# The four-token sums of the first half batch, computed by GpSimd between its weight pieces in place of VectorE

## What is computed

```python
B, H, S, D = 4, 8, 576, 64
q_d = q.reshape(B, H, S // 4, 4, D).mean(axis=3)      # likewise k_d, v_d
out_up = np.repeat(softmax_attention(q_d, k_d, v_d), 4, axis=2)
scores = where(abs(i - j) < 4, (q @ k.T) / 8, -1e9)
out_local = softmax(scores) @ v
x = (out_up + out_local)  # as 2304 tokens x 512
h = x @ w_in              # 512 -> 2048
x = where(h > 0, h, exp(min(h, 0)) - 1) @ w_out       # 2048 -> 512
g = x @ w_gate            # 512 -> 1536
out = (g * sigmoid(g) * (x @ w_val)) @ w_out2
```

## Time and profile before

| | us |
|---|---|
| three runs | 1067.14, 1067.51, 1065.35 |
| median | 1067.14 |
| span of the profiled execution | 1064.6 |
| TensorE busy in it | 1020.6 (96%) |
| VectorE, ScalarE, GpSimd busy in it | 492.5, 383.6, 179.7 |

### The profile page before, as it was taken

The page is one execution under the profiler, slowest core; times in us unless marked ns, Lnnn a source line. Parts: engine busy times, 40 slices in busy tenths (PEclk is TensorE's granted clock), DMA queues, the critical chain, the costliest instruction groups (busy, mean ns, idle before and its releaser), DMA issues.

```text
span 1064.6 us, 20019 instructions
## 1 busy us (share of the span) xinstructions
PE 1020.6 (96%) x7136; PEld 990.1 (93%) x7136; DVE 492.5 (46%) x1459; ACT 383.6 (36%) x1204; POOL 179.7 (17%) x207
## 2 busy tenths in 40 slices
PE   5499999899999999999999999999999999999998
PEld 4389999799998899999999999999999999999998
DVE  7856576365674555755644333223223232232222
ACT  5645344254453444545435622212212221221212
POOL 4740331001331012410007720000000000000000
PEclk9999999899999899999999999999999999999999
DMA  7621021111211111211034611000000001000000
GB/s 234 205 70 42 29 90 38 47 47 30 65 60 29 50 47 53 68 29 47 10 96 139 174 57 31 30 1 30 32 1 30 30 1 31 30 1 1 31 1 31
DMA packets 35146, 54.96 MB, mean 52 GB/s; under 512 B 3488, under 2 KB 23136, under 8 KB 35040
## 3 DMA queue, kind: packets, MB, share of 16 engines
q1 hardware_dynamic: 35040, 53.55, 16.7%
HBM read 44.10 MB, written 9.44 MB: 50 GB/s over the span
## 4 chain that ended last, share of the span: by engine, by line
PE 85%; DVE 6%; ACT 3%; issue 3%; DMA 1%; POOL 0%; SPq 0%; DVEq 0%; ACTq 0%
PE bank L314 26%; PE bank L315 25%; PE bank L316 25%; PE bank L274 3%; PE bank L300 2%; PE bank L285 1%; DVE g_sb L558 1%; PE bank L279 1%; PE bank L306 1%; ACT weights L704 1%; DVE prob L524 1%; DVE neg_max L509 1%; DVE v_pool L433 1%; DVE g_sb L560 1%; DVE prob L505 1%
## 5 line engine op out<-in xcount | busy, mean ns | idle before, releaser
L314 PE MATMUL bank<-x_hl,weights 128*128 128x384 f32 (+1 forms) x1088 | 352.1, 324 | 10.1 <-issue 9.6
L315 PE MATMUL bank<-x_hl,weights 128*128 128x384 f32 (+1 forms) x1088 | 347.5, 319 | 0.0
L316 PE MATMUL bank<-x_hl,weights 128*128 128x384 f32 (+1 forms) x1088 | 347.4, 319 | 0.0
L314 PEld LDWEIGHTS bank<-x_hl,weights 128*128 128x128 f32 x1088 | 206.2, 190 | 9.9 <-issue 8.7
L315 PEld LDWEIGHTS bank<-x_hl,weights 128*128 128x128 f32 x1088 | 206.5, 190 | 6.1 <-issue 6.1
L316 PEld LDWEIGHTS bank<-x_hl,weights 128*128 128x128 f32 x1088 | 206.3, 190 | 0.0
L314 PE MATMUL bank<-g_hl,weights 128*128 128x288 f32 x512 | 158.3, 309 | 1.5 <-DVE g_hl L566 1.5
L315 PE MATMUL bank<-g_hl,weights 128*128 128x288 f32 x512 | 152.7, 298 | 0.0
L316 PE MATMUL bank<-g_hl,weights 128*128 128x288 f32 x512 | 152.4, 298 | 0.0
L594 DVE TENSOR_TENSOR u_sb<-bank,u_sb 128x384 f32<-128x384 f32 x72 | 40.1, 557 | 199.3 <-ACT u_sb L744 199.3
L566 DVE TENSOR_TENSOR g_hl<-g_sb,g_hl 128x288 fp32r<-128x288 f32 x128 | 71.9, 562 | 86.6 <-ACT g_hl L681 86.6
(11 more groups left out here) (71 smaller groups left out, 1281.6 us busy)
## 6 DMA issues: line engine op xcount, KB each, us to landing
late_stages<-w SPq DMA_DIRECT2D x31, 256.0 KB, 3.2
v_win<-v_windows SPq DMA_DIRECT2D x32, 153.0 KB
q_sb<-qT SPq DMA_DIRECT2D x32, 144.0 KB, 2.2
k_sb<-kT SPq DMA_DIRECT2D x16, 288.0 KB, 3.0
v_raw<-v_rows SPq DMA_DIRECT2D x16, 288.0 KB
yT_scratch<-y_sb SPq DMA_DIRECT2D x32, 144.0 KB, 1.9
y_raw<-yT_scratch SPq DMA_DIRECT2D x6, 768.0 KB, 4.5
outT<-out_sb SPq DMA_DIRECT2D x24, 192.0 KB, 1.9
```

The lines of the kernel that those rows point to most:

```text
L314: nc.tensor.matmul(bank[:, 0:n_cols], w_hi, x_hi, start=first, stop=False)
L315: nc.tensor.matmul(bank[:, 0:n_cols], w_hi, x_lo, start=False, stop=False)
L316: return nc.tensor.matmul(bank[:, 0:n_cols], w_lo, x_hi, start=False, stop=last)
```

## The change

All sums of half 0 of batch 0, and those of the queries of the first pair of half 1, go from VectorE to GpSimd, between its weight pieces in the rhythm in which ScalarE takes them. `x_low` stays with VectorE there. Nothing is changed in the loop, and TensorE, ScalarE and SyncE keep their instructions and their order. The semaphore counts of the halving additions are shifted by one batch, as the sums of batch 0 now count too.

```diff
@@ sum_tokens' counts in pool_k, pool_q, pool_v
-                       (a - 1) * PAIRS + pair + 1).then_inc(k_pooled, 1)
+                       a * PAIRS + pair + 1).then_inc(k_pooled, 1)
...
-                       q_half_sums, halves(a, h, PAIRS) + pair - PAIRS).then_inc(q_pooled, 1)
+                       q_half_sums, halves(a, h, PAIRS) + pair + 1).then_inc(q_pooled, 1)
...
-        def attention_extras(eng, math, a, h, u, final=False):
+        def attention_x_low(eng, math, a, h, u):
+
+            if USES[u][0] == "T" and u and USES[u - 1][0] == "O":
+                x_low(eng, math, a, h, USES[u - 1][1])
+            if u == NU - 1:
+                x_low(eng, math, a, h, PAIRS - 1)
+
+        def attention_sums(eng, math, a, h, u, final=False):
...
+        def attention_extras(eng, math, a, h, u, final=False):
+
+            attention_sums(eng, math, a, h, u, final)
+            attention_x_low(eng, math, a, h, u)
...
@@ VectorE
-            pool_qk(dve, nc.vector, 0, 0, 0)
             for u in range(NU):
                 dve_attention(dve, 0, 0, u, att_all)
-                attention_extras(dve, nc.vector, 0, 0, u)
+                attention_x_low(dve, nc.vector, 0, 0, u)
...
@@ GpSimd
-            for n in range(N_PIECES_A):
+            pool_qk(pool, nc.gpsimd, 0, 0, 0)
+            for u in range(NU):
+                attention_sums(pool, nc.gpsimd, 0, 0, u)
+                for n in range(u * SPLIT_BEFORE // NU, (u + 1) * SPLIT_BEFORE // NU):
+                    pool_weight_low(pool, n, n, stage_a(n)[0])
+            for n in range(SPLIT_BEFORE, N_PIECES_A):
                 pool_weight_low(pool, n, n, stage_a(n)[0])
```

More of the change, by code:

```diff
@@ L463, in pool_v @@
             sum_tokens(eng, math, v_pool[:, pair, :, :], x, x[..., 0:2], v_half_sums,
-                       (a - 1) * PAIRS + pair + 1).then_inc(v_pooled, 1)
+                       a * PAIRS + pair + 1).then_inc(v_pooled, 1)
         def pool_qk(eng, math, a, h, pair):
```

## The result

The changed kernel takes 1071.35 us (median of 18 runs, 1068.14 to 1073.61) beside 1066.06 us for the kernel before in the same comparison (18 runs, 1062.50 to 1070.13). The ratio is 1.0047, with a 95% interval of 1.0036 to 1.0059: some 5 us slower. The profiled executions stand at spans of 1070.1 and 1064.6 us.

A forecast was written before the change was run, and what follows sets the result against it. TensorE bounds the kernel from 74 us, so only the prologue counts: GpSimd's 28th weight piece moves ScalarE's first high part by 4.6 us, the clock returns 1.5, net +3.1 on 1067.14, giving 1070.2 us; range 1066.8 to 1073.0.

The forecast's parts named there:

- the slow clock stays: Rival, 24%: TensorE's pace falls again before the second accumulation or stays slow longer, nothing comes back: +4.6 us, 1071.7.
- GpSimd's queue: Prologue: pieces, sums, conflicts and idle time end GpSimd's 28th weight piece at 64.9, moving ScalarE's first high part by 4.6 us.
- Those waits cost nothing as long as that distance stands: Prologue: VectorE's longer conflict waits, up to 2.04 us, are free, since its side is ready at about 58, before 64.9.
- the high part waits for VectorE again: Sign of being wrong: ScalarE's first high part at the prologue's end is released by VectorE, not by GpSimd's 28th piece.
- The rule of the skill: VectorE operations with two SBUF inputs need the port pair shared with GpSimd, locked for a whole instruction; `tensor_reduce` never does.
- The clock: TensorE's slow stretch falls at 66.0 to 70.5, the pause shrinks from 2.1 to 0.5 us, and 1.5 us comes back.
- Behind it TensorE sets the time: From 74 us on TensorE is busy all the time, so prologue gains or losses reach the end one for one.
- Faster: Rival, 7%: GpSimd's idle time takes the sums in, VectorE's relief shortens the prologue; 1063.5 if sums cost VectorE's price.
- The decision point: The gate stays at 60.3 if GpSimd's sums behind 9.03 cost 13.8 us instead of 18.4; everything below is gain.

The follow-up runs named there:

- the wait behind the values sums: The changed kernel, with GpSimd waiting for the end of its own values sum before the next weight piece: 1069.99 us against 1066.46, ratio 1.0039.
- the small additions: The kernel before, with four small additions into unread scratch in GpSimd's queue: 1068.03 us on 72 partitions, 1062.72 on 128, 1069.31 on 112.

## Why the prediction was right or wrong

The direction was right and the size near: +3.1 us was forecast with 0.72 for slower, and about 5 us came, with the median inside the range. The reason given was the second of two. In the changed kernel another loss of nearly the same size stood ahead of it, so that the number was met in part by luck. The rival "the slow clock stays" (+4.6, 1071.7) came even closer in number, and it did not hold the lock-out either.

- **GpSimd's queue** was right. 64.9 was the sum for the 28th piece. It was 64.53 with the wait behind the values sums, and 65.57 in the changed kernel, where 2.4 us of waiting for ScalarE (1.40 and 1.05) are in it. The sum had no such waiting, and the prediction had named it as a sign of being wrong. Ahead of the first of the two ScalarE itself had waited 9.7 us for VectorE. Sums took what the earlier trace rows say, or a little less (values 1.95 to 1.97 and 0.72 to 0.83).
- **"Those waits cost nothing as long as that distance stands"** is the step that failed. I priced VectorE's waits at no more than one instruction of GpSimd, "up to the 2.04 us of a values addition". Two of them were 4.42 and 9.29 us. VectorE's side was ready at 66.2, not at 58; the prediction's own sentence had named that distance as the cover, and it was gone. Even with the wait behind the values sums it was ready only at 60.2, and the hidden units started at 54.99, not 3 us ahead of 55.16: the ordinary waits alone ate nearly all of VectorE's relief. It had named "the high part waits for VectorE again" as what would show it wrong, and so it was.
- Every row of before had conflicts in which GpSimd used all 128 partitions, or had nothing queued behind a values sum. The rule of the skill and the rows agreed on that, and I carried it over to a case neither had. No rival of mine held the lock-out.
- **The clock** was wrong. I expected 1.5 us back. The slow stretch of the kernel before, too, was 3.41 us by the granted clock (69.96 to 73.37), shorter than I had read it from the matmuls. In the changed kernel the pause ahead of the first scores stayed at 2.14 us, because the whole chain had moved with VectorE, and the granted clock was 0.5 for 6.83 us behind it, where it was 3.41 us before. The stretch behind the pause at the first repeat of the loop, at 205 and 211, was shorter by as much (3.4 us, 6.8 before), so that the clock gave and took nothing in all. Even with the wait behind the values sums, where the pause was 3.71 us as I had it in kind, the clock was at 0.5 from 64.69 for 10.24 us and the first scores came at 74.78, not 73.65: TensorE itself was too slow to be ready.
- **"Behind it TensorE sets the time"** holds roughly. From 75 to 205 us TensorE was busy for 125.0 us of 130 and not all the time; a shift of 6.0 us at 75 was one of 5.5 in the spans.
- **Faster** was given 7%. Its reasoning is borne out by other kernels: with fewer sums on GpSimd, VectorE's relief does shorten the prologue, and those with queries and keys show it at 2 to 2.5 us, in intervals that only just leave out no change. The decision point, 13.8 us of sums, was not tried itself. With two values sums fewer, 18.4 - 2 x 2.9 = 12.6 us of them, the prediction's sum gives 59.1 for the 28th piece; it ended at 59.74, and the time was that of the kernel before.

## What to carry to other kernels

Work moved to GpSimd had two prices here besides its duration: the gate at the end of GpSimd's own queue, and what VectorE waits at the ports they share. Look at the number of partitions of every GpSimd instruction that has others queued behind it; where it isn't 128, let GpSimd wait for that instruction before the next one. With the values alone on GpSimd that was worth 10 us, and the time was that of the kernel before again. And when a loss has the predicted size, still look at who released the wait: two causes that moved the high part by 4 and 6 us lay behind one another here, and mending the first alone brought little.

## What the runs showed of the hardware

- Behind a GpSimd instruction on 72 or 112 partitions, a VectorE operation with two inputs in SBUF, or a multiplication by a scalar there, was held for 3.6 to 9.3 us, through up to seven further GpSimd instructions. It ended each time when GpSimd's run ended or it took up a sum or one of the small additions. Behind the same instruction on 128 partitions it was not.
- VectorE's reductions and its operations that read PSUM took no longer in any of these runs than in the kernel before (the values reductions 1.97 us at most, L535, L543 in the changed kernel, 0.46 throughout). Few of them were issued behind such an instruction of GpSimd, though, since they stood in the queue behind the operation that was held.
- A TensorE pause at one place can return as a slow stretch of 3.41, 6.83 or 10.24 us behind it. The kernel before varies with it too: of its 19 runs beside the first experiments the fastest, at 1063.07 us, had a mean granted clock of 0.994 and the slowest, at 1070.27, one of 0.990. A change of 2 us in the prologue has to be timed against that.
